# Token mixing of an attention, feed-forward and mixer kernel: products up and down in another order, and other times for the weight reads

## What is computed

```python
h = np.maximum(xt @ w_tok1, 0.0) @ w_tok2     # xt = x transposed, tokens 576 -> 256 -> 576, for each of 512 features
u = x + h.transpose(0, 2, 1)
h2 = np.maximum(u @ w_ch1, 0.0) @ w_ch2       # features 512 -> 1536 -> 512
return (u + h2).astype(np.float32)
```

## Time and profile before

| | |
|---|---|
| median of 3 runs | 689.85 us (688.78 to 692.72) |
| the profiled execution | 692.18 us |
| its span, first to last instruction | 690.4 us |
| PE busy | 663.2 us, 96% |
| DVE busy | 510.0 us, 74% |
| ACT busy | 319.3 us, 46% |
| POOL busy | 255.2 us, 37% |
| mean granted TensorE clock | 0.982 |

### The profile page before, as it was taken

One profiled execution on the slowest core, in us unless ns is written; L12 is line 12 of the kernel. 1 busy time (PEld: TensorE's weight loads), 2 busy tenths in 40 slices (PEclk: granted clock), 3 DMA queues, 4 the chain that ended last, 5 costly groups with the idle time before them and its releaser, 6 DMA issues.

```text
span 690.4 us, 17219 instructions
## 1 busy us (share of the span) xinstructions
PE 663.2 (96%) x6977; PEld 639.5 (93%) x6977; DVE 510.0 (74%) x853; ACT 319.3 (46%) x676; POOL 255.2 (37%) x318
## 2 busy tenths in 40 slices
PE   8999999999999999999969798999999899999997
PEld 7878999999999999989958698999999899999997
DVE  5469868686777768786875669887887799676763
ACT  4375562625444452626434216654546656343440
POOL 6474664846464554725478420000001111111000
PEclk9799999999999999999989899999999999999999
DMA  9861343232432332297495053567659998979784
GB/s 201 223 192 28 62 80 81 44 66 52 104 52 49 61 76 58 61 142 155 138 221 191 9 197 121 181 226 244 210 205 318 359 359 263 312 194 310 206 224 68
DMA packets 204926, 109.46 MB, mean 159 GB/s; under 512 B 163112, under 2 KB 192944, under 8 KB 204336
## 3 DMA queue, kind: packets, MB, share of 16 engines
q1 hardware_dynamic: 187888, 64.66, 37.3%
q0 software_dynamic: 7008, 38.41, 16.6%
q10 hardware_dynamic: 9952, 5.31, 3.3%
HBM read 69.41 MB, written 38.93 MB: 157 GB/s over the span
## 4 chain that ended last, share of the span: by engine, by line
PE 85%; DVE 7%; DMA 3%; issue 2%; ACT 1%; SPq 1%; POOL 0%; DVEq 0%; POOLq 0%; ACTq 0%
PE bank L967 9%; PE bank L969 8%; PE bank L968 8%; PE tq L967 3%; PE tq L968 3%; PE tq L969 3%; DMA h_rows<-hq 3%; PE bank L1586 3%; PE bank L1587 3%; PE bank L1588 3%; PE bank L843 3%; PE bank L1022 3%; PE bank L1818 3%; PE bank L1820 3%; PE bank L1819 3%; PE s L631 2%
## 5 line engine op out<-in xcount | busy, mean ns | idle before, releaser
L1778 ACT ACTIVATE ck__hi<-ck__raw 128x576 fp32r<-128x576 f32 x84 | 51.4, 675 | 64.4 <-DMA ck__raw<-h_rows 64.4
L1782 DVE TENSOR_TENSOR ck__lo<-ck__raw,ck__hi 128x576 fp32r<-128x576 f32 x84 | 59.5, 748 | 14.6 <-ACT ck__hi L1778 14.6
L1754 POOL DMA_DIRECT2D ck__raw<-h_rows x28 | 14.9, 534 | 145.5 <-PE bank L1588 49.2
L1062 POOL TENSOR_TENSOR k_lo<-kr,k_hi 128x288 fp32r<-128x288 f32 x64 | 55.2, 866 | 27.2 <-ACT k_hi L1058 27.0
L1104 DVE RECIPROCAL rg<-rg 128x288 f32<-128x288 f32 x32 | 61.5, 1923 | 0.0
L1586 PE MATMUL bank<-U__hi,W__hi 128*128 128x288 f32 x192 | 57.1, 297 | 3.9 <-ACT hq L1618 3.4
L1587 PE MATMUL bank<-U__hi,W__lo 128*128 128x288 f32 x192 | 56.6, 295 | 0.0
L1588 PE MATMUL bank<-U__lo,W__hi 128*128 128x288 f32 x192 | 56.5, 294 | 0.0
L967 PE MATMUL bank<-k_hi,WV_hi 128*128 128x288 f32 x184 | 55.5, 301 | 0.0
L968 PE MATMUL bank<-k_hi,WV_lo 128*128 128x288 f32 x184 | 54.3, 295 | 0.0
L969 PE MATMUL bank<-k_lo,WV_hi 128*128 128x288 f32 x184 | 54.1, 294 | 0.0
(11 more groups left out here) (273 smaller groups left out, 2352.4 us busy)
## 6 DMA issues: line engine op xcount, KB each, us to landing
h_rows<-hq SPq DMA_DIRECT2D x24, 1008.0 KB, 5.5
ck__raw<-h_rows POOLq DMA_DIRECT2D x28, 864.0 KB, 5.9
x_turned<-xblocks SPq DMA_DIRECT2D x16, 288.0 KB, 5.1
u_kept<-X SPq DMA_DIRECT2D x4, 1152.0 KB, 4.7
W__raw<-in_moe_w_ch POOLq DMA_DIRECT2D x6, 768.0 KB, 7.6
ub<-u_kept POOLq DMA_DIRECT2D x4, 1152.0 KB, 8.5
out_x<-ob SPq DMA_DIRECT2D x56, 72.0 KB, 5.0
vt<-in_v SPq DMA_DIRECT2D x70, 48.0 KB
```

The costliest lines, as they stand in the source:

```text
L1062: e.tensor_tensor(lo, t, hi.bitcast(F32), ALU.subtract).then_inc(Z.lo_done, 1)
L1782: e.tensor_tensor(lo, raw, hi.bitcast(F32), ALU.subtract).then_inc(Z.cl_done, 1)
```

## The change

It does six things.

1. Token mixing goes one batch ahead. PE's order is up(0), up(1), down(0), up(2), down(1), up(3), down(2), down(3). For that, `token_up` gives its PE part and its ACT and DVE part as two steps, h1 has two buffers, the results up take turns in four PSUM banks of their own and the results down in four others, `first_token_down` goes, and xT of batch 2 gets its own place.
2. The first slice of w_ch1 is read from the end of the feed-forward's last up product on, its sums and a part of its splits stand at the end of the feed-forward; the other two slices' reads and splits move too. w_tok1's split is in three pieces and stands later in the feed-forward, w_tok2's split is in the token stage.
3. x_in of batches 2 and 3 goes from POOL's queue to SP's.
4. The second slice's lows (L1509) stand between the adds of batch 3.
5. The late reads of w_ch2 and h_rows are spread: each waits for its own count of steps, where three or two started together.
6. In the last three chunks all products of the first row of tiles come before those of the second, and each row is added and transposed on its own.

```diff
-        xTs = [xT0, xT1, xT0, xT3]
+        xT2, _ = weights("xT2", [P, NTT * DM], U0)
+        xTs = [xT0, xT1, xT2, xT3]
...
-        h1, _ = split("h1", [P, 2 * DM], U1)
+        h1s = [split(f"h1_{i}", [P, 2 * DM], off)[0] for i, off in enumerate((U1, XT0))]
...
-        work = [s2[:, 0:512], s2[:, 512:1024], bank[6][:, :], bank[7][:, :]]
+        h_banks = [s2[:, 0:512], s2[:, 512:1024], tq2[:, 0:512], tq2[:, 512:1024]]
+        row_banks = [bank[0][:, 0:HALF], bank[1][:, 0:HALF], bank[6][:, 0:HALF], bank[7][:, 0:HALF]]
...
-        pieces2 = [parts(T1, P, 0, 4 * TOK), parts(T1, P, 4 * TOK, TOK), parts(T2, P, 0, 2 * S)]
+        pieces2 = [parts(T1, P, 0, 2 * TOK), parts(T1, P, 2 * TOK, 2 * TOK), parts(T1, P, 4 * TOK, TOK), parts(T2, P, 0, 2 * S)]
...
                 elif b == 2:
-                    e.wait_ge(Z.t1p_done, 2)
+                    e.wait_ge(Z.mm_done, HP * NU)
...
-            return dict(sync=queue) if b < 2 else dict(gpsimd=queue)
+            return dict(sync=queue)
...
+        def h_bank_free(e, b):
+
+            if b == 0:
+                e.wait_ge(Z.x_done, ND)
+            elif b == 1:
+                e.wait_ge(Z.x2_done, DT * NU)
+            else:
+                e.wait_ge(Z.h1l_done, 2 * (b - 1))
...
+                if b > 1:
+                    e.wait_ge(Z.t2p_done, 8 * (b - 1))
+                e.activation(h1[0][:, c], ps, ACT.Relu).then_inc(Z.h1h_done, 1)
...
+            return dict(tensor=tensor), dict(scalar=scalar, vector=vector)
...
+                if i == 0:
+                    e.wait_ge(Z.h1l_done, 2 * (b + 1))
+                    e.wait_ge(Z.tw_lo, N_T)
+                if 8 * b + i < 4:
+                    e.wait_ge(Z.x2_done, DT * NU)
+                else:
+                    e.wait_ge(Z.u_done, 8 * b + i - 3)
...
                 if s == 0:
-                    e.wait_ge(Z.mm_done, HP * NU - DT)
-                    e.wait_ge(Z.lo_done, FT1 * NU)
+                    e.wait_ge(Z.mm_done, HP * NU - 2 * DT)
...
                 elif part == 3:
+                    e.wait_ge(Z.p4_done, NQ - 3)
                     e.dma_start(tiles(W2[S3][2][:, :], NJ), w2_block(1, 0)).then_inc(Z.w2_in3, 16)
+                elif part == 4:
+                    e.wait_ge(Z.p4_done, NQ - 1)
                     e.dma_start(tiles(a11_again[:, :], NJ), w2_block(0, 0)).then_inc(Z.w2_in3, 16)
...
                 if n < 2:
-                    e.wait_ge(Z.p4_done, NJ * (B - 1))
+                    e.wait_ge(Z.p4_done, NJ * (B - 1) + n)
                 elif n < NCK:
-                    e.wait_ge(Z.p4_done, NQ - 2)
+                    e.wait_ge(Z.p4_done, NQ - 2 + 2 * (n - 2))
...
+        def down_last():
+
+            chunks = range(21 * B - 3, 21 * B)
+
+            def tensor(e):
+                for g in chunks:
+                    e.wait_ge(Z.cl_done, g + 1)
+                    first = down_part(e, g, 0)
+                first.then_inc(Z.first_done, 1)
+                for g in chunks:
+                    down_part(e, g, 1).then_inc(Z.chunk_done, 1)
+            return dict(tensor=tensor)
...
-            ff[-9].append(load_w1(0))
...
-            ff[-12].append(load_second_token_weights())
+            ff[-13] += [load_w1(0), load_second_token_weights()]
             ff[-10].append(x_in(1))
-            for i in range(N_T):
-                ff[2 * i - 25 if i < N_T - 1 else -8].append(split_token_weights(i))
+            for i, (hi, lo) in enumerate(tw):
+                ff[i - 18].append(hi)
+                ff[i - 16].append(lo)
             for i, x in enumerate(xs):
-                ff[2 * i - 14].append(x)
+                ff[2 * i - 13].append(x)
+            ff[-9] += [w1_sum(0, k) for k in range(4)]
+            ff[-4] += [w1_parts(0, i)[0] for i in range(7)]
+            ff[-2] += [w1_parts(0, i)[1] for i in range(3)]
...
+            steps = products(0) + products(1) + [x_in(2)] + [x_blocks(3, d) for d in range(DT)] + [x_out(3), x_in(3)]
+            steps += [x_parts(1, i) for i in range(NTT)] + [tw_hi, tw_lo, h(0, 0)] + los(w1[0])[3:] + [h(0, 1)]
+            steps += [x_parts(2, i) for i in range(NTT)] + [h(1, 0), h(1, 1)]
+            steps += rows[0] + [keep_u(0)] + products(2) + [x_parts(3, i) for i in range(NTT)] + [h(2, 0), h(2, 1)]
+            steps += rows[1] + [keep_u(1), load_w1(1)] + products(3) + [u_sum(0, k) for k in range(4)]
+            steps += his(u0) + los(u0) + [h(3, 0), h(3, 1)]
+            steps += rows[2] + [load_w1(2), keep_u(2)] + [w1_sum(1, k) for k in range(4)] + his(w1[1])
+            for i, step in enumerate(rows[3]):
+                steps += [step] + los(w1[1])[i:i + 1]
...
-            extra[23] += [load_h(3)] + [chunk_parts(g) for g in range(3, 6)]
-            extra[24] += [load_u(0), load_w2(4), w2_parts(A12)]
+            extra[23] += [load_w2(4)] + [chunk_parts(g) for g in range(3, 6)]
+            extra[24] += [load_u(0), load_h(3), w2_parts(A12)]
...
-                if g == 3:
-                    steps.append(load_w2(5))
+                if g in (3, 6):
+                    steps.append(load_w2({3: 5, 6: 6}[g]))
...
-                if g in (1, 6):
-                    steps.append(w2_sum({1: S3, 6: S4}[g]))
-                elif g in (3, 9, 13):
-                    steps.append(w2_parts({3: S3, 9: S4, 13: A22}[g]))
+                if g in (2, 8):
+                    steps.append(w2_sum({2: S3, 8: S4}[g]))
+                elif g in (4, 10, 14):
+                    steps.append(w2_parts({4: S3, 10: S4, 14: A22}[g]))
```

More of the change, by code:

```diff
@@ L1391, in tensor @@
                             c0 = TOK * (NTT - 1) + P * m_
-                            e.matmul(work_bank(b, m_), T1[w][r, c0:c0 + P], xT[x][r, t0:t0 + DM], start=i == 0, stop=False)
+                            e.matmul(h_bank(b, m_), T1[w][r, c0:c0 + P], xT[x][r, t0:t0 + DM], start=i == 0, stop=False)
                 product(e, ps, T1, cols(TOK, P * m, P), xT, cols(DM, 0, DM), range(NTT - 1), start=False,
@@ L1419, in vector @@
                 e.tensor_tensor(x, ps, x, ALU.add).then_inc(Z.u_done, 1)
[L1420 to L1435 removed]
+            return dict(tensor=tensor, vector=vector)
         def token_rows(b):
[L1438 removed]
+            return [token_down(b, t, d) for t in range(2) for d in range(DT)]
         def keep_u(b):
@@ L1798, in down_free, with down_part @@
             e.wait_ge(Z.added, 14 * b_ + 2 * i_ + d + 1)
+        def down_part(e, g, d):
+            b, i, k = g // 21, g // 3 % 7, g % 3
+            onto = i not in (0, 1, 3)
+            xh, xl = chunk(g, 0), chunk(g, 1)
+            wh, wl = W2[i][:2]
+            ps = down_bank(b, i, d)
+            if k == 0:
+                down_free(e, b, i, d)
+            for m in range(2):
+                w = slice(2 * P * (2 * k + m) + P * d, 2 * P * (2 * k + m) + P * (d + 1))
+                x = slice(HALF * m, HALF * (m + 1))
+                e.matmul(ps, wh[:, w], xh[:, x], start=not onto and k == 0 and m == 0, stop=False, skip_group_check=onto)
+                e.matmul(ps, wl[:, w], xh[:, x], start=False, stop=False, skip_group_check=onto)
+                last = e.matmul(ps, wh[:, w], xl[:, x], start=False, stop=k == 2 and m == 1, skip_group_check=onto)
+            return last
         def down_chunk(g):
             b, i, k = g // 21, g // 3 % 7, g % 3
-            xh, xl = chunk(g, 0), chunk(g, 1)
-            wh, wl = W2[i][:2]
             def tensor(e):
-                onto = i not in (0, 1, 3)
                 e.wait_ge(Z.cl_done, g + 1)
@@ L1810, in tensor, with add_down @@
                     e.wait_ge(Z.w2_lo, i + 1)
-                for d in range(2):
-                    ps = down_bank(b, i, d)
-                    if k == 0:
-                        down_free(e, b, i, d)
-                    for m in range(2):
-                        w = slice(2 * P * (2 * k + m) + P * d, 2 * P * (2 * k + m) + P * (d + 1))
-                        x = slice(HALF * m, HALF * (m + 1))
-                        e.matmul(ps, wh[:, w], xh[:, x], start=not onto and k == 0 and m == 0, stop=False, skip_group_check=onto)
-                        e.matmul(ps, wl[:, w], xh[:, x], start=False, stop=False, skip_group_check=onto)
-                        last = e.matmul(ps, wh[:, w], xl[:, x], start=False, stop=k == 2 and m == 1, skip_group_check=onto)
-                    if d:
-                        last.then_inc(Z.chunk_done, 1)
-                    elif k == 2:
-                        last.then_inc(Z.first_done, 1)
+                first = down_part(e, g, 0)
+                if k == 2:
+                    first.then_inc(Z.first_done, 1)
[6 more added lines that the diff above has]
+                    e.wait_ge(Z.cl_done, g + 1)
+                    first = down_part(e, g, 0)
+                first.then_inc(Z.first_done, 1)
+                for g in chunks:
+                    down_part(e, g, 1).then_inc(Z.chunk_done, 1)
             return dict(tensor=tensor)
```

(16 more changed lines are left out.)

85 lines of the change are left out of this document (28 added, 57 removed).

## The result

The changed kernel took 667.32 us (median of 4 runs, 665.99 to 668.09) against 691.29 for the kernel before (4 runs, 688.78 to 695.12). The ratio is 0.965, with a 95% interval of 0.960 to 0.970. The forecast was 667.6. Of its terms one was met, two were too small and two too large, and a part of the hit is chance, as will be seen.

What follows compares the result with a forecast made beforehand. PE, busy 96% of the span, was taken as the bound, so only its waits and slow clock could be won. Terms of 15.4, 2.3, 1.4, 3.4 and 1.0 sum to 23.5; forecast 667.6 us, between 668.7 and 666.4, range 663.0 to 676.0.

Steps and rivals of the forecast that it cites:

- Part 1: Token mixing: running one batch ahead removes the two long waits and the slow clock behind them, 15.4 us won.
- The given-back 0.5: Token mixing, down(2): a stall for DVE's U lows and first add, 0 to 5.3 us possible, 0.5 taken.
- price of a batch: Token mixing: an undisturbed batch takes PE 6.57 us up and 6.66 down, 13.23 together.
- Down(0)'s slack of 1.4: Token mixing, batch 0: DVE's h_lo is ready at 352.2, 1.4 us before down(0) starts at 353.6.
- Part 2: Feed-forward: T1's split moved to where no reciprocal stands removes PE's waits, 1.4 us won.
- Part 3: Queues: moving issues of 2 us each off POOL, which is not waited for there, wins 0.
- Part 4: Start of the up stage: W lows made between down(3)'s adds remove PE's wait for DVE, 2.3 us won, bounds 0 and 2.3.
- Part 5: End of the up stage: spread late reads remove waits for ACT's copy, 3.4 us won; likely down-stage cost 0, bound about 5.
- The sum by bytes: Late h_rows stores: with one read beside it, 1872 KB would take 7.1 us instead of 10.4 for 2736 KB.
- The second rival: Down stage: W_5 or W_6 late, chunk lows behind them; price 1.2 to 5, 669 to 673 us, chance 0.10.
- Part 6: Kernel end: the first row's stores are out earlier, so the last issue ends 0.96 us sooner; 1.0 won, bounds 0 and 1.
- The other rivals: Token mixing: DVE bound, 673 to 678, chance 0.14; xT late, 671 to 677, 0.08; SP's queue late, 695, 0.04.

Runs made afterwards that it cites:

- u_lows: The changed kernel with the last four lows of the second W slice behind batch 3's adds again, not between them: 674.28 us, ratio 0.976.
- v_sum: The changed kernel with one line moved, DVE's sums of W_5 behind chunk 8's adds instead of ahead of them: 667.37 us, ratio 0.968.
- after_again: The changed kernel run once more, unchanged, in a later set: 668.96 us, ratio 0.970.
- after_third: The changed kernel run a third time, unchanged, in another set: 667.85 us, ratio 0.968.
- u_end: The changed kernel with both rows in each of the last three chunks and both adds and transposes at the end again: 668.94 us, ratio 0.969.
- p_beside: The changed kernel with seven more POOL additions while DVE makes the lows of U: 673.05 us, ratio 0.973.
- v_best: The changed kernel with W_5's sums behind chunk 8's adds, two W lows behind batch 0's adds, four last stores on ACT: 666.03 us, ratio 0.963.
- b_reads: The kernel before with only the late reads spread and W_4 to W_6's sums and splits one or two chunks later: 690.19 us, ratio 0.998.

## Why the prediction was right, and where it was not

**Part 1, -15.4: measured -17.0.** The mechanism held. The given-back 0.5 at the fifth result of down(2) didn't come: the lows of U took 0.70 each, beside a quiet POOL, and ended at 372.8, one microsecond before down(2) began. The step that was mis-sized is the price of a batch, 13.23. The changed kernel's batches take 6.57 up and 6.41 down on average (26.3 and 25.6 us for four), where the prediction had 6.57 and 6.66; that is 1.0 for four batches, beside the 0.5 that wasn't given back. The predicted slots were 340.4, 347.0, 353.6 and so on; shifted by 5.8, each is met within 0.5 us up to down(2). Down(0)'s slack of 1.4 was too kind. It was 0.8 in the first profile (h_lo ends at 346.86), and in the two others PE waited 0.8 and 0.7 there, since DVE began its four W lows 1.1 us later in the stage (7.7 and 7.5 us into it instead of 6.5) and took 5.8 us for them beside POOL instead of 5.2.

**Part 2, -1.4: measured -2.0.** The term was read off the list of waits. The block of 96 products in which the waits stand took 14.68 us and takes 12.79 now, 1.9 less: the stops cost PE 0.5 more than the 1.4 of waits that are listed. No run undoes this part alone, nor Part 3.

**Part 4, -2.3: measured -2.3**, and 1.3 of slow clock on top in u_lows, none in the kernel before.

**Part 5, -3.4 with a likely cost of 0: measured about 0.** This is the step that failed. The gain came in some executions only. In the first profile it did: the stores landed in 7.3 to 8.9 us where 10.4 stood in the earlier trace rows. The sum by bytes, 7.1 us, doesn't hold: with one read beside it a store took up to 11.6, and over all profiles the copy's wait falls from 3.0 to 1.2, which is 1.8 won and not 3.4. Above all the cost was not 0. The prediction said: "If DVE's queue decided, which has the same work ahead either way, nothing changes." DVE's queue did decide, and it does have the same work ahead, but it stands still in the midst of it, for reads that land later. And the place that counts isn't chunk 15 and W_5's lows, but chunk 12, whose bank is free only after chunk 8's adds. DVE in the changed kernel (idle before an instruction and its releaser in brackets):

```profile
534.94 1.43 DVE L1776 TENSOR_TENSOR ck__lo<-ck__raw,ck__hi 128x576 fp32r<-128x576 f32 x2 [1.04 <-ACT ck__hi L1772]
536.28 0.82 DVE L1858 TENSOR_TENSOR ub<-bank,ub 128x288 f32<-128x288 f32 x2
537.01 1.42 DVE L1776 TENSOR_TENSOR ck__lo<-ck__raw,ck__hi 128x576 fp32r<-128x576 f32 x2
539.17 1.76 DVE L1704 TENSOR_TENSOR W__raw<-W__raw,W__hi 128x1536 f32<-128x1536 f32 x1 [0.74 <-DMA W__raw<-in_moe_w_ch]
540.96 1.76 DVE L1706 TENSOR_TENSOR W__raw<-W__raw,W__lo 128x1536 f32<-128x1536 f32 x1
542.64 0.75 DVE L1776 TENSOR_TENSOR ck__lo<-ck__raw,ck__hi 128x576 fp32r<-128x576 f32 x1
543.31 0.82 DVE L1858 TENSOR_TENSOR ub<-s,ub 128x288 f32<-128x288 f32 x2
```

The same adds in the kernel before:

```profile
569.03 0.82 DVE L1846 TENSOR_TENSOR ub<-s,ub 128x288 f32<-128x288 f32 x2
```

The adds of the last row, for chunk 8, begin 543.31 - 522.64 = 20.7 us into the down stage; before they began at 18.1 (569.03 - 550.94). PE wanted them at 19.4 (541.99). DVE did the same work ahead of them in both. Of the 2.6 us, 2.3 are three pauses of DVE that the kernel before doesn't have: 0.54 for ub's read (at 530.74), which was issued as early as before and took 7.6 us instead of 6.0, and 1.04 and 0.74 for reads of h_rows and w_ch2 that are issued later than before. v_sum shows that another order mends it. And the wait cost more than itself:

```profile
543.90 0.37 PE L1806 MATMUL s<-ck__hi,W__hi 128*128 128x288 f32 x1 [1.91 <-DVE ub L1858]
544.00:547.00 3.00, 3.00 (x18) 3.00 (x19) 3.00 (x4) 2.48 (x5) 0.00 (x0) 0.72 1.01 425
```

The down stage is 3.65 longer than before: 1.9 of wait; 1.5 of clock, since without its wait it is that much above the 134.4 to 134.5 that after_again, after_third, u_end and p_beside have without theirs; and some 0.2 that those have too against the kernel before (134.2). The second rival was this one, with its price (1.2 to 5) but the wrong chunk, and it has come on top of the forecast's mechanism, not instead of it.

**Part 6, -1.0: measured -0.4.** ACT's last issue did come 0.9 nearer to the last matmul. But the row that is turned one step earlier leaves its stores with SP, which was done after ACT:

```profile
661.33 0.48 DVE L1867 STREAM_TRANSPOSE ob<-ub 128x288 f32<-128x288 f32 x1
659.82 2.88 ACTq L1881 DMA_DIRECT2D out_x<-ob  x3
659.88 3.77 SPq L1881 DMA_DIRECT2D out_x<-ob  x7
```

ACT is through at 662.70, SP at 663.65. The prediction read one of two queues. v_best, in which ACT takes four of SP's stores, has the rest of the 1.0.

**The sum.** 23.5 was forecast and 21.2 measured in this pair of profiles (17.0 + 2.0 + 5.5 - 3.7 + 0.4, the up stage's 5.5 being Part 4 and the gain of Part 5). The prediction added the terms to an execution of 692.18 and knew that it lay 2.3 above the median, "and I do not know where". Most likely it lay in the slow clock of 20 to 30 us: b_reads, the same program up to there, kept 1.00 and reached the first product of xT at 337.77, 2.7 earlier. With the base put half way, 667.6, the surplus of the sum (2.3) and what was left of that slow clock in the base nearly cancelled. So a part of the hit is luck: the same kernel gave 668.96 and 667.85 in the next sets, and its gain there is 21.1 and 22.9.

The other rivals: xT was not late (up(2) and up(3) began in their slots), and SP's queue was not: x_in(3) was issued at 348.3, 19 us ahead of up(3).

## What to carry to other kernels

Find what a wait hangs on in the other engine's order before adding slack: two reordered lists of small instructions gave 12 of these 17 us, and the batch ahead, with what was moved for it, gave the other 5. When reads are moved later, count the pauses that they put into each engine that consumes them, and look for the next place where PE wants a bank back, not only for the tile that is read. Before adding terms to one profiled execution, compare its granted clock stretch by stretch with a second one's.
